# A fused attention and mixture-of-experts kernel: four of nine causal masks issued one block later, and two activations moved behind two casts

## The reference

```python
scores = scale * np.matmul(q, k.transpose(0, 1, 3, 2))
cum = np.cumsum(np.log(np.clip(f, 0.0001, 1.0)), axis=-1)
scores = np.where(causal, -1e9, scores + cum[..., :, None] - cum[..., None, :])
attn = softmax(scores); x = attn @ v            # 2304 tokens x 512
h = x @ w_in                                    # 512 -> 2048
g = np.where(h >= 1, h, np.where(h <= -1, 0.0, (h + 1) ** 2 / 4))
y = g @ w_out                                   # 2048 -> 512
e = argmax over 8 experts of cosine(y, expert_emb) / tau
out = gate * (np.maximum(y @ w1[e], 0) @ w2[e])
```

## Time and profile before

| what | value |
|---|---|
| median of 3 runs | 864.99 us (860.3 to 865.04) |
| the profiled execution | 864.53 us, its span 862.4 us |
| attention, from the page and the timeline | about 9 to 217 us of the span |
| one pair in the steady part | 12.35 us |
| granted TensorE clock, mean | 0.994 |
| PE busy in the span | 98% |
| DVE, ACT, POOL busy in the span | 49%, 46%, 42% |

### The profile page before, as it was taken

One profiled execution on the slowest core, in us unless ns is written; L12 is line 12 of the kernel. 1 busy time (PEld: TensorE's weight loads), 2 busy tenths in 40 slices (PEclk: granted clock), 3 DMA queues, 4 the chain that ended last, 5 costly groups with the idle time before them and its releaser, 6 DMA issues.

```text
span 862.4 us, 13820 instructions
## 1 busy us (share of the span) xinstructions
PE 841.0 (98%) x5050; PEld 786.2 (91%) x5051; DVE 420.5 (49%) x1002; ACT 398.6 (46%) x915; POOL 363.3 (42%) x366
## 2 busy tenths in 40 slices
PE   7899999999999999999999999999999999999996
PEld 5788888889999999999999999999998998998985
DVE  5777888887654544444445445455535210211201
ACT  5677777777666534534443544443332111111211
POOL 5666788884565311102201111074411492010285
PEclk8999999999999999999999999999999999999999
DMA  6467788883200211021021022342233354213041
GB/s 204 152 204 237 224 271 261 258 264 87 56 1 1 84 46 55 25 100 35 27 101 56 29 101 62 116 136 66 67 99 98 111 170 136 67 55 123 22 138 42
DMA packets 66334, 94.58 MB, mean 110 GB/s; under 512 B 6662, under 2 KB 42502, under 8 KB 66256
## 3 DMA queue, kind: packets, MB, share of 16 engines
q1 hardware_dynamic: 58016, 78.84, 30.1%
q10 hardware_dynamic: 6480, 10.03, 3.3%
q0 software_dynamic: 1760, 4.72, 1.4%
HBM read 69.82 MB, written 24.27 MB: 109 GB/s over the span
## 4 chain that ended last, share of the span: by engine, by line
PE 79%; DVE 9%; ACT 5%; issue 5%; DMA 1%; POOL 0%; SPq 0%; DVEq 0%; POOLq 0%; ACTq 0%
PE psum L1454 24%; PE psum L1456 24%; PE psum L1455 24%; DVE pr L1063 3%; ACT pth L828 3%; DVE ptl L1085 3%; PE psum L1408 2%; ACT pr L818 2%; PE psum L1383 2%; DVE rden L1069 1%; PE psum L1425 1%; DVE xl L1106 1%; PE psum L1537 1%; PE psum L1521 0%; PE psum L1522 0%
## 5 line engine op out<-in xcount | busy, mean ns | idle before, releaser
L1454 PE MATMUL psum<-xh,winh 128*128 128x384 f32 x384 | 129.1, 336 | 0.0
L1454 PE MATMUL psum<-gh,wouth 128*128 128x384 f32 x384 | 128.3, 334 | 0.2 <-issue 0.2
L1455 PE MATMUL psum<-xl,winh 128*128 128x384 f32 x384 | 128.4, 334 | 0.0
L1456 PE MATMUL psum<-xh,winl 128*128 128x384 f32 x384 | 128.4, 334 | 0.0
L1456 PE MATMUL psum<-gh,woutl 128*128 128x384 f32 x384 | 128.3, 334 | 0.0
L1455 PE MATMUL psum<-gl,wouth 128*128 128x384 f32 x384 | 128.3, 334 | 0.0
L852 ACT ACTIVATE hpos<-psum,minus 128x384 f32<-128x384 f32 x96 | 55.9, 582 | 142.2 <-DVE hclip L1111 142.0
L1116 DVE TENSOR_TENSOR g<-hpos,hsq 128x384 f32<-128x384 f32 x96 | 65.6, 684 | 109.2 <-ACT hsq L854 109.2
L818 ACT ACTIVATE pr<-pr,mmin 128x64 f32<-128x64 f32 (+2 forms) x144 | 81.5, 566 | 46.4 <-DVE mmin L1063 46.4
L649 POOL TENSOR_TENSOR xst<-xst 128x384 f32<-128x384 f32 x24 | 24.6, 1024 | 175.7 <-DMA xst<-rinv_d 175.7
L1217 DVE SCALAR_TENSOR_TENSOR hl<-psum,hh 128x384 fp32r<-128x384 f32 x48 | 26.8, 557 | 139.5 <-ACT hh L905 139.5
(11 more groups left out here) (230 smaller groups left out, 1911.6 us busy)
## 6 DMA issues: line engine op xcount, KB each, us to landing
praw<-moe_w SPq DMA_DIRECT2D x48, 256.0 KB, 2.7
qraw<-q SPq DMA_DIRECT2D x15, 576.0 KB, 5.8
vraw<-vk SPq DMA_DIRECT2D x16, 320.0 KB, 3.4
xh<-yh_d SPq DMA_DIRECT2D x20, 256.0 KB, 4.0
xl<-yl_d SPq DMA_DIRECT2D x20, 256.0 KB, 4.3
kraw<-k SPq DMA_DIRECT2D x16, 288.0 KB, 4.6
c<-cum_d SPq DMA_DIRECT2D x32, 144.0 KB, 4.2
xa_d<-xo SPq DMA_DIRECT2D x16, 288.0 KB, 3.8
```

Of the source, the lines that this page charges most:

```text
L1454: nc.tensor.matmul(psum_at, ah, bh, start=start, stop=False)
L1455: nc.tensor.matmul(psum_at, ah, bl, start=False, stop=False)
L1456: return nc.tensor.matmul(psum_at, al, bh, start=False, stop=stop)
```

## The change

Masks of blocks 1, 4, 6 and 8 of each pair are issued behind the products of the next block, just ahead of that block's own mask (for block 8: behind the products of block 0 of the next pair). The very last block of all keeps its place. The number of products and their order within a PSUM bank are as before, and the signals `scored` come in the same order. On ScalarE `rise(0)` is issued one step later, behind `high` of the last block.

```diff
-                if n == STEPS - 1:
+                if n == STEPS:
                     rise(0)
...
+            MASK_LATER = (1, 4, 6, 8)
+
+            def mask(n):
+                p, i = tile_of(n)
+                bank, w = (10 * p + i) % 4, keys(i)
+                if i == NB - 1:
+                    bank, w = bank + 1, w // 2
+                nc.tensor.matmul(psum[:, bank, w - D:w], ident_b[:], mask_b[:], start=False,
+                                 stop=True).then_inc(scored, 1)
...
-                    dst = psum[:, bank, w - D:w]
...
-                    dst = psum[:, bank + 1, w // 2 - D:w // 2]
-                nc.tensor.matmul(dst, ident_b[:], mask_b[:], start=False, stop=True).then_inc(scored, 1)
+                if i in MASK_LATER and n + 1 < STEPS:
+                    return
+                if n >= 1 and (i - 1) % NB in MASK_LATER:
+                    mask(n - 1)
+                mask(n)
```

## The result

The changed kernel takes 879.60 us (median of 4 runs, 878.51 to 880.03), the kernel before 863.11 us in the same comparison (860.30 to 865.04). The ratio is 1.0184, 95% interval 1.0158 to 1.0209: **slower by 16 us**, where 883.5 and a range of 873 to 891 were forecast.

A forecast was written before the change was run, and what follows sets the result against it. The prediction took each attention pair to be bound by a chain of waits through DVE, ACT and PE, without PE's products. To 864.5 us it added 14.0 + 0.6 + 5.3 - 0.9 = 19.0, giving 883.5 us, range 873 to 891.

The forecast's parts named there:

- The lateness of the masks: In attention, block 8's later mask makes `pr` 8 1.00 us late; pairs 1 to 14 lose 14.0 us, the last 0.6.
- The second mask of two in a row: On PE, a mask standing directly behind another was taken to cost 0.06 us, between 0.04 and 0.12.
- PE's products are not in the chain.: In an attention pair, PE's products do not bound the time, except through when they are ready; saved PE work shortens nothing.
- The collision: In eight pairs loading x, GpSimd's `ql` would catch VectorE's `xl`, making `pr` 8 another 0.66 us late: 5.3 us.
- The end: At the end of attention, the last casts come sooner with `rise(0)` moved: 0.9 us won, between 0 and 1.1.
- From pair 0 to pair 1: Stretch from `pr` 8 of the first pair to that of the next: 1.00 us longer from the late mask.
- The sum: Whole kernel: 14.0 + 0.6 + 5.3 - 0.9 = 19.0 us slower, giving 883.5 us.
- The signs: Expected in the changed profile: pairs of 13.3 to 13.5 us, later near 14.0; PE idle nearly 1 us more; `xl` over 2.
- No collision: Rival: in pairs loading x, `xl` still gets in before `ql`, or `ql` waits for other input; 878 us, chance 0.25.
- The feedback by way of the x load: Rival: late `xl` delays the next x, hence `ql` and the next `xl`, or the clock falls; 885 to 893, chance 0.08.
- the three slower cases: Whole-kernel outcomes above 873.6 us: the forecast itself 0.56, no collision 0.25, self-feeding delay 0.08; given together as 0.88.

The follow-up runs named there:

- The 0.22 us at block 7: Kernel before with the first pass of block 7 done twice, an extra overwritten product per pair: 868.83 us against 864.20, ratio 1.0053.
- the 11.98 us pairs: Pairs without x in the kernel before with `rise(0)`, attend_late_a, `turn` 2, cast 1 and `xl` moved; 867.39 us against 864.75.
- the last two experiments: Kernel before reordered on TensorE and ScalarE, `rise(0)` moved, `xl` in step 5: ratio 1.0029; same with `xl` one place earlier: 1.0022.

## Why the prediction was right, point by point

- *The lateness of the masks.* Shown. The step said that `pr` 8 would be 1.00 us late and that nothing behind it has slack. It comes 0.98 us later behind the two transposes and starts 0.24 us behind the mask, and the pair is 0.93 us longer with masks alone, 1.04 with block 8 alone, and no longer with blocks 1 and 4. The missing 0.05 us is slack behind `pr` 8: in pair 3 before, exp 8 ended at 61.20 and the cast behind it started at 61.30; in the changed kernel it starts as exp 8 ends. The second mask of two in a row costs about 0.03 us, not the 0.06 I took.
- *"PE's products are not in the chain."* **Wrong.** The 0.22 us at block 7 came through whole in the kernel before. There TensorE works without a break from `turn` 0, and both casts on the way start 0.67 us behind its transposes: the cast behind `turn` 1 (57.73 and 58.40) and the one behind `turn` 2 (134.76 is 0.04 us behind the mask at 134.72, and the cast is at 135.43). The exps end no more than 0.1 us ahead of them, so two chains of nearly equal length meet at each cast, and in the pairs without x TensorE's is the longer at both. I saw ScalarE idle for one of them and did not ask what else would be late. That it did not hurt the forecast is luck of this change: it lengthens the first chain by 1 us, and that the second got 0.17 us shorter is then worth nothing. Where nothing is late, savings on TensorE are real, by these rows up to the 0.1 us that the exps end sooner, and beyond that only with the exps sooner too: the 11.98 us pairs shortened both.
- *The collision.* Shown: `xl` is 2.3 to 2.4 us long and ends 0.4 us behind `ql`, and away from `ql` it is 0.55 and the pairs are 0.55 us shorter on average. Its size was over: 0.51 us per pair beyond the masks, not 0.66. And it has a sister that I did not price, `rden`, by the rows worth 0.4 us a pair with block 6 alone.
- *The end.* Shown, 1.1 us for 0.9; its bound was 1.1.
- *From pair 0 to pair 1* the forecast had 1.00 us and the table has 0.34. The lateness is there in full; the two profiles of the table each lose time to the clock in or just before this stretch, the one before more (last section). At full clock it is 13.20 us with late masks against 12.23 without, +0.97.
- *The sum.* 19.0 forecast, 16.0 measured: 1.2 us of the difference is the collision's size, 0.9 the masks in pairs 2 to 14, 0.7 the way from pair 0 to 1, 0.2 the end. The 879.6 us lie just under the 880 to 888 that the bounds of the terms gave.
- *The signs.* All came but two sizes. TensorE's idle time ahead of the eight transposes grew from 0.04 to 0.61 us in pair 3, not by nearly 1 us; about 0.5 us more of it stands earlier, ahead of block 2's products. Pairs with x took 13.8 us, not near 14.0.
- *The rivals.* "No collision" had the nearest time, 878, and is refuted by `xl` at 2.35 us: a time alone would have picked the wrong case. The feedback by way of the x load did not happen in the changed kernel, but it is what held up the last two experiments. The chances of the three slower cases add to 0.89, not 0.88.

## What to carry to other kernels

A signal moved behind other work is priced at who waits for it, not at the instruction. An engine that idles ahead of an instruction shows one chain into it; before calling the other inputs free, look how long they had been ready, or lengthen them by a known amount and see whether it comes through. When one engine is made late, list what it will now meet on the engines that it shares something with.

## What the hardware showed that was not expected

The kernel before takes 860 to 867 us in the same comparison; on one chip 10 of its 23 executions took 860.2 to 860.6 us and 13 took 863.9 to 866.9. The profiles show where such a difference arises. The kernel before from 13 to 20 us (after a stretch in which PE idled 1.74 us for DVE at 10.9), and the kernel with more work at block 3:

```profile
13.00:20.00 7.00, 7.00 (x29) 5.33 (x29) 3.49 (x14) 4.05 (x17) 6.28 (x17) 0.51 0.58 172
```

```profile
13.00:20.00 7.00, 6.41 (x48) 5.26 (x49) 5.30 (x23) 5.30 (x20) 6.68 (x18) 1.00 0.59 167
```

In the first the granted clock is 0.51, the lower of the two levels (1.2 GHz), and PE gets through 29 matmuls; in the second it is 1.00 and PE gets through 48. `pr` 8 of the first pair starts at 21.07 in the one and 19.11 in the other. That is the 2 us of the first line of the table. Kernels with late masks show both: 19.09 to 19.37 in three profiles, 21.23 to 21.93 in three.

The slow start has a second price, at full clock. From there to `pr` 8 of pair 1 the kernel before takes 13.86 us and the other 12.23. VectorE comes late, and its `rden` falls just behind the start of `ql` (24.28, 2.64 us):

```profile
24.38 2.57 DVE L1069 TENSOR_SCALAR rden<-rsum 128x9 f32<-128x9 f32 x1
```

In the other it takes 0.52 us. The profiles with only `rise(0)` moved and with masks 1 and 4 show the slow start too, and the same behind it: `rden` 2.48 and 2.57 us, 13.77 and 13.86 us to pair 1. Together the two make 3.6 us, most of the distance between the groups. The changed kernel's profile had the clock up from 13 to 20 us; it fell to 0.50 for 3.4 us at 21.9, with TensorE idle since 20.9 for `ptl`, and the eight transposes there took 1.60 us to the next product instead of 0.82. Its 14.20 us to pair 1 are 1.0 us more than the 13.20 of the kernel with the masks alone, whose clock is full there. Executions of the same kernel fall on one or the other side, so that a difference of 2 to 4 us between two single executions says nothing here.
